# Expert slots: h turned by 32x32 block transposes over a DRAM exchange, second products two slots behind

## The chip, the core and the metric

One core of one Trainium2 chip runs the kernel in one launch. The metric is device time in microseconds (us), the median of the runs. The core has five engines with queues of their own: TensorE (matrix products and transposes, results in PSUM), VectorE, ScalarE, GpSimd and SyncE (SP), which here only issues DMA transfers. Engines wait for one another by semaphores.

## The reference

Attention with a cumulative bias gives x [4 x 576, 512]. Then comes the part that the change touches, a mixture of 8 experts with one expert per token, and a gated feed-forward layer with a short convolution.

```
logits = x @ w_gate;  e = argmax(logits)            # or the expert of the token before
h   = maximum(x[b, s] @ w1[e], 0.0)                 # 512 -> 1024
y   = p[e] * (h @ w2[e])                            # 1024 -> 512
h2  = maximum(y @ w_in, 0);  conv over 3 tokens;  out = (h2 * sigmoid(conv)) @ w_out
```

## The kernel before

`attention` runs first and takes about the first 200 us. A routing stage (`tensor_route`, `vector_route`, 200 to 219 us) sorts the 2304 tokens by expert into SLOTS = 25 slots of 128 tokens, each slot with tokens of one expert only. In this run the experts have 3, 2, 3, 3, 3, 2, 3 and the rest of the slots. Then the expert stage works slot by slot, from 219 to 529 us, and the last stage (w_in, convolution, w_out) follows.

Every product is taken in three parts, high x high, high x low and low x high (`PARTS`), where high is the value rounded to fp32r and low is what it leaves. So a slot's first product `hidden(s)` is 2 halves of 4 blocks of 3 parts, 24 matrix products on TensorE (L1289), into `h_bank` (wide_bank0, one PSUM bank for each half). The second, `output(s)`, is 8 blocks of 3 parts, 24 products too (L1306), into `y_bank` (row_bank0). An operand must have the summed dimension on the partitions. Hence x of the slot is turned by 4 TensorE transposes (`turn_x`, L1255) and moved from PSUM into high and low (`move_x`, VectorE, L1374 and L1376), and h is cut at zero (`relu`, L1382, into `h_sb`), turned by 8 TensorE transposes into `ht_bank` (wide_bank1; `turn_h`, L1327) and moved likewise into `h_tr` (`move_h`, L1392 and L1396). `move_y` (L1411) copies y to `y_sb`, and SP stores it to `y_sorted` in DRAM (L1206). There is one `y_bank`, one `h_sb`, one `xs_tr`, one `h_tr`, one `ht_bank`, and the semaphores guard them.

The order is written out by hand. TensorE's loop body is

```
hidden(s);  turn_x(s + 1);  output(s - 1);  turn_h(s)
```

and VectorE's is relu(s), move_x(s + 1), move_y(s - 1), move_h(s). The last slot is cut in halves: hidden(24, first half), output(23), turn_last, turn_h(24, first half), hidden(24, second half), output(24). `turn_last` makes 5 small transposes for placing the last slot's rows. Before a slot's products TensorE loads two numbers of the slot into registers (`weights_of`, L1271 and L1272): which half of the weight ring, and how many low parts must be ready.

The weight ring holds two experts. ScalarE issues the load of w1 of expert e when the first products of e - 2 are done, makes the high parts (L902), then issues w2 when the second products of e - 2 are done, and makes its high parts. GpSimd makes the low parts (L912) behind them. Before that, GpSimd gathers the rows of x of all 25 slots by indirect DMAs (L1164), two in flight.

## Time and profile before

| | us |
|---|---|
| median of 3 runs | 746.98 |
| lowest, highest | 746.82, 748.25 |
| span of the profiled execution | 746.1 |
| TensorE busy in it | 735.4 |
| VectorE busy in it | 432.8 |
| GpSimd busy | 329.1 |
| ScalarE busy | 322.1 |

The page of the profile gives the busy time of each engine, the load of each in 40 slices of 18.65 us, and the chain of work that ended last. The timeline merges like instructions in order of time. A row has the start and the length in us, then engine, line, operation, what it writes and reads, and the count; in brackets stands how long the engine was idle before it and what ended that. A matrix product's start is recorded, its end is modelled. A product's length (0.39 us) is therefore longer than the distance between two starts.

### The profile page before, as it was taken

The numbers are of one execution on the slowest core, as the hardware profiler recorded it, in microseconds if no ns is written. First come the engines' busy times: TensorE is split into PE (matmuls) and PEld (weight loads), VectorE is DVE, ScalarE is ACT, GpSimd is POOL, SyncE is SP. The second block draws the span as 40 slices with busy tenths as digits, with TensorE's granted clock in tenths as the row PEclk, the third lists the DMA queues.
The fourth block names the chain that finished last, engine by engine and source line by source line (L and its number), as shares of the span: only waits on it lengthen the run. The fifth ranks groups of instructions, "written<-read, shape, count | busy, mean of one in ns | idle before, by whom it ended". The sixth has DMA issues, their size and how long they took to land.

```text
span 746.1 us, 15123 instructions
## 1 busy us (share of the span) xinstructions
PE 735.4 (99%) x4971; PEld 626.7 (84%) x4971; DVE 432.8 (58%) x1042; ACT 322.1 (43%) x635; POOL 329.1 (44%) x442
## 2 busy tenths in 40 slices
PE   8999999999989999999999999999999999999998
PEld 6788887887887888888888888888899889889986
DVE  5777878878776544444444545454399455636510
ACT  5777878878430112212121311100397345535620
POOL 7759788887325469444444854400521100000000
PEclk9999999999999999999999999999999999999999
DMA  7888879984064666333334543200421110000011
GB/s 161 206 211 224 230 204 217 239 223 124 17 200 142 232 193 249 144 127 142 127 141 127 171 160 119 89 29 29 139 62 33 43 36 15 29 29 14 29 43 56
DMA packets 99848, 93.39 MB, mean 125 GB/s; under 512 B 62124, under 2 KB 71620, under 8 KB 99780
## 3 DMA queue, kind: packets, MB, share of 16 engines
q1 hardware_dynamic: 79252, 46.51, 22.9%
q10 hardware_dynamic: 17056, 34.69, 13.6%
q0 software_dynamic: 3472, 11.28, 5.3%
q8 instruction: 44, 0.72, 0.4%
q14 instruction: 24, 0.20, 0.1%
HBM read 76.13 MB, written 16.33 MB: 124 GB/s over the span
## 4 chain that ended last, share of the span: by engine, by line
PE 70%; DVE 1%; DMA 0%; issue 0%; ACT 0%; POOLq 0%; DVEq 0%; ACTq 0%
PE row_bank L1306 19%; PE wide_bank L1289 18%; PE wide_bank L1551 14%; PE row_bank L1589 13%; PE wide_bank L1327 3%; PE bank L1255 1%; PE bank L1520 1%; DMA x_slots<-x_rows,token_of 0%; PE bank L1540 0%; PE wide_bank L28 0%; PE row_bank L1540 0%; PE bank L1017 0%; DVE y_sb L1411 0%; DVE xs_tr L1376 0%; DVE xs_tr L1374 0%
## 5 line engine op out<-in xcount | busy, mean ns | idle before, releaser
L912 POOL TENSOR_TENSOR ring<-raw_w,ring 128x2048 fp32r<-128x2048 f32 x28 | 128.6, 4614 | 87.7 <-ACT ring L902 87.7
L1289 PE MATMUL wide_bank<-ring,xs_tr 128*128 x600 | 143.3, 394 | 0.7 <-DVE xs_tr L1368 0.4
L1306 PE MATMUL row_bank<-ring,h_tr 128*128 x600 | 143.5, 394 | 0.0
L902 ACT ACTIVATE ring<-raw_w 128x2048 fp32r<-128x2048 f32 x30 | 55.8, 1908 | 200.3 <-DMA raw_w<-in_moe_w_dram 169.6
L1306 PEld LDWEIGHTS row_bank<-ring,h_tr 128*128 128x128 f32 x600 | 110.8, 188 | 22.7
L1289 PEld LDWEIGHTS wide_bank<-ring,xs_tr 128*128 128x128 f32 x600 | 110.7, 188 | 22.9 <-issue 1.1
L1551 PE MATMUL wide_bank<-x_tr,ring 128*128 128x288 f32 x768 | 107.7, 297 | 0.0
L1551 PEld LDWEIGHTS wide_bank<-x_tr,ring 128*128 128x128 f32 x768 | 103.2, 188 | 0.9
L1589 PE MATMUL row_bank<-ring,g_tr 128*128 128x512 f32 x432 | 100.1, 389 | 0.0
L1589 PEld LDWEIGHTS row_bank<-ring,g_tr 128*128 128x128 f32 x432 | 80.5, 188 | 16.1
L692 ACT ACTIVATE prob<-score,row_min 128x128 f32<-128x128 f32 (+2 forms) x144 | 83.4, 580 | 17.9 <-DVE row_min L555 14.6
L251 POOL TENSOR_SCALAR bias<-ncum_row,cum_col 128x128 f32<-128x128 f32 (+3 forms) x128 | 67.2, 535 | 37.1 <-DVE row_min L555 31.9
L1641 DVE SCALAR_TENSOR_TENSOR conv<-h_pad,conv_col,conv 128x576 f32<-128x576 f32 x64 | 52.2, 816 | 53.9 <-ACT conv L1702 52.7
L555 DVE CUSTOM_DVE_ANT_0 score<-score_ps,bias 128x128 f32<-128x128 f32 (+2 forms) x144 | 69.2, 514 | 19.2 <-issue 13.3
L1411 DVE COPY y_sb<-row_bank 128x512 f32<-128x512 f32 x25 | 17.3, 694 | 98.8 <-PE row_bank L1306 98.8
L1382 DVE TENSOR_SCALAR h_sb<-wide_bank 128x512 f32<-128x512 f32 x48 | 33.2, 691 | 56.7 <-PE wide_bank L1289 56.0
L1493 POOL DMA_INDIRECT y_tok<-y_sorted,place_i x20 | 20.2, 1010 | 92.9 <-PE bank L1520 46.4
L361 PE MATMUL turn_ps<-identity,prob 128*128 128x128 f32 x320 | 50.1, 279 | 1.0 <-ACT tail_tr L709 0.6
L1164 POOL DMA_INDIRECT x_slots<-x_rows,token_of x25 | 26.0, 1041 | 49.1 <-DMA x_slots<-x_rows,token_of 24.1
L361 PEld LDWEIGHTS turn_ps<-identity,prob 128*128 128x128 f32 x320 | 36.4, 141 | 11.6 <-issue 5.0
L321 PE MATMUL score_ps<-k_tr,q_tr 64*128 64x128 f32 (+3 forms) x256 | 44.9, 469 | 0.1
L1693 ACT ACTIVATE h_pad<-wide_bank 128x576 f32<-128x576 f32 x32 | 20.9, 654 | 55.6 <-PE wide_bank L1551 55.5
(236 smaller groups left out, 1009.5 us busy)
## 6 DMA issues: line engine op xcount, KB each, us to landing
raw_w<-in_moe_w_dram ACTq DMA_DIRECT2D x12, 2048.0 KB, 8.8
ncum_row<-cum_rows SPq DMA_DIRECT2D x15, 512.0 KB, 5.6
y_sorted<-y_sb SPq DMA_DIRECT2D x26, 256.0 KB
raw_w<-in_moe_w_dram SPq DMA_DIRECT2D x12, 512.0 KB, 3.9
ncum_tail<-cum_rows SPq DMA_DIRECT2D x32, 144.0 KB, 4.4
out_dram<-out_sb ACTq DMA_DIRECT2D x18, 256.0 KB, 2.0
v_nat<-in_v_dram SPq DMA_DIRECT2D x32, 128.0 KB, 3.0
q_nat<-in_q_dram SPq DMA_DIRECT2D x30, 128.0 KB, 4.0
```

Source lines behind the costliest of these rows:

```text
L251: return nc.gpsimd.tensor_scalar(out, row, col, 1.0, ALU.add, ALU.mult)
L321: nc.tensor.matmul(out[:, hh, 0:(i + 1) * P], q_tr[u][at, i * P:(i + 1) * P], k_tr[u][at, 0:(i + 1) * P], start=True, stop=True).then_inc( ...
L361: last = nc.tensor.transpose(bank[:, at + j * P:at + (j + 1) * P], prob[unit(p, n) % 4][:, j * P:(j + 1) * P], identity[:, :])
L555: nc.vector.tensor_tensor_reduce(out=o, in0=a, in1=b, scale=1.0, scalar=3.0e38, op0=ALU.add, op1=ALU.min, accum_out=row_min[:, at % 4:at % ...
L692: nc.scalar.activation(prob[at % 4][:, 0:w], score[at % 3][:, 0:w], ACT.Exp, bias=row_min[:, at % 4:at % 4 + 1], scale=-1.0, accum_out=row ...
L902: nc.scalar.activation(high, whole, ACT.Copy).then_inc(high_ready, 1)
L912: nc.gpsimd.tensor_tensor(low, whole, high.bitcast(F32), ALU.subtract).then_inc(low_ready, 1)
L1289: last = nc.tensor.matmul(h_bank[:, half, :], xs_tr[:, a, kb, :], ring[:, bass.ds(n, 1), b, at:at + FH].rearrange("p a c -> p (a c)"), sta ...
L1306: last = nc.tensor.matmul(y_bank[:, :], h_tr[:, a, kb, :], ring[:, bass.ds(n, 1), 2 + b, kb * D:(kb + 1) * D].rearrange("p a c -> p (a c)" ...
L1551: last = nc.tensor.matmul(wide_bank[j % 2][:, half, 0:HALF], ring[:, 0, w, col:col + P], x2_tr[:, x, kb, at:at + HALF], start=kb == 0 and ...
L1589: last = nc.tensor.matmul(row_bank[outs % 2][:, :], g_tr[:, a, kb, lo:hi], ring[:, 0, 2 + w, kb * D:(kb + 1) * D], start=kb == 0 and (a, w ...
L1641: ins = V.scalar_tensor_tensor(c[:, :], h[:, k:k + S], conv_col[:, k * KF + f:k * KF + f + 1], c[:, :], ALU.mult, ALU.add)
```

## The change

Slots 2 to 23 are no longer turned by TensorE. VectorE's relu writes h to `h_sb` with the columns ordered so that each quarter of them (32 of every 128) lies together. SP writes `h_sb` to DRAM (`h_turn`), waits for it, and reads it back in four transfers, each of which takes one quarter of the columns to one quarter of the partitions, with the 128 tokens side by side (`h_exchange`). The buffer read into is `x_slots` of slots 0 to 3, used by then. VectorE turns the 32x32 blocks from there to `ht_bank` (`h_turned`), and makes high and low parts out of PSUM (`move_h_blocks`). Slots 0, 1 and 24 are turned by TensorE as before.

The second products run two slots behind the first. In the loop TensorE does hidden(s), turn_x(s + 1), output(s - 2). In four places the order differs: slots 2, 3 and 4 at the start, and the end. Each slot has a second need number of its own for w2, for which `vector_route` gets four more steps. ScalarE and GpSimd take the weights interleaved: w1 of e + 1, then w2 of e. Four gathers of x may be in flight. VectorE's, ScalarE's, GpSimd's and SP's loops are written out.

```diff
         nc.gpsimd.tensor_tensor(low, whole, high.bitcast(F32), ALU.subtract).then_inc(low_ready, 1)
 
-    def low_parts(pool, e, n):
...
+    def parts_upto(e, piece):
+        if e < 2:
+            return PIECES * e + piece + 1
+        if piece >= PIECES // 2:
+            return PIECES * e + PIECES - 1 + piece - (e == E) * (PIECES // 2)
+        return PIECES * e - 1 + piece + (e == 2) * (PIECES // 2)
+
+    def low_parts(pool, e, w):
+
+        for piece in (2 * w, 2 * w + 1):
+            low_part(pool, e, piece)
 
...
-        act.wait_ge(first_loaded[n], 16)
+        act.wait_ge(first_loaded[n // 2], 16 * (n % 2 + 1))
...
+            if part % 2:
+                sp.wait_ge(first_loaded[part // 2], 16)
...
+        then(V.tensor_scalar(slot_f[:, 3, :], slot_f[:, 1, :], 3.0, -float(PIECES // 2), ALU.is_ge, ALU.mult))
+        then(V.tensor_scalar(slot_f[:, 4, :], slot_f[:, 1, :], 2.0, float(PIECES // 2), ALU.is_ge, ALU.mult))
+        then(V.tensor_scalar(slot_f[:, 2, :], slot_f[:, 1, :], float(PIECES), float(PIECES), ALU.mult, ALU.add))
         then(V.tensor_scalar(slot_f[:, 1, :], slot_f[:, 1, :], float(PIECES), float(PIECES // 2), ALU.mult, ALU.add))
+        then(V.tensor_tensor(slot_f[:, 1:3, :], slot_f[:, 1:3, :], slot_f[:, 3:5, :], ALU.add))
         then(V.tensor_copy(free_i[:, :], tiles_upto[0:1, 1:1 + E]))
         dve.wait_ge(exps_ready, 1)
-        V.tensor_copy(slot_i[:, :, :], slot_f[:, :, :]).then_inc(slot_ready, 1)
+        V.tensor_copy(slot_i[:, :, :], slot_f[:, 0:3, :]).then_inc(slot_ready, 1)
...
-            above(pool, slot_loaded[s % 2], 16 * (s // 2))
+            above(pool, slot_loaded[s % GATHERS], 16 * (s // GATHERS))
             pool.indirect_dma_start(out=x_slots[:, s, :], out_offset=None, in_=x_rows,
-                                    in_offset=bass.IndirectOffsetOnAxis(ap=token_of[:, s:s + 1], axis=0)).then_inc(slot_loaded[s % 2], 16)
+                                    in_offset=bass.IndirectOffsetOnAxis(ap=token_of[:, s:s + 1], axis=0)).then_inc(slot_loaded[s % GATHERS], 16)
...
+    BY_PE = 2
+    h_swapped = [x_slots[:, 2 * n:2 * n + 2, :].rearrange("p s d -> p (s d)") for n in range(2)]
+    h_out, h_back, h_blocks, y_begun = sem("h_out"), sem("h_back"), sem("h_blocks"), sem("y_begun")
...
+    Q = 32
+    QUARTERS = P // Q
...
     def sync_experts(sp):
         sp.wait_ge(y_zero, 1)
         sp.dma_start(y_sorted[LAST:LAST + P, :], y_sb[:, :]).then_inc(last_zeroed, 16)
-        with sp.Fori(0, SLOTS - 1) as s:
+
+        def h_exchange(s):
+            n, i = s % 2, s - BY_PE
+            sp.wait_ge(h_ready, 2 * s + 2)
+            above(sp, h_back, 16 * QUARTERS * i)
+            sp.dma_start(h_turn[n], h_sb[:, :]).then_inc(h_out, 16)
+            sp.wait_ge(h_out, 16 * (i + 1))
+            if i >= 2:
+                sp.wait_ge(h_blocks, 2 * i - 2)
+            for g in range(QUARTERS):
+                sp.dma_start(h_swapped[n][g * Q:(g + 1) * Q, :].rearrange("p (i c) -> p i c", i=QUARTERS),
+                             h_turn[n][:, g * F // QUARTERS:(g + 1) * F // QUARTERS].rearrange("(i r) c -> r i c", r=Q))\
+                    .then_inc(h_back, 16)
+
+        def y_store(s):
             sp.wait_ge(y_ready, s + 1)
-            sp.dma_start(y_sorted[bass.ds(s * P, P), :], y_sb[:, :]).then_inc(y_stored, 16)
+            sp.dma_start(y_sorted[s * P:(s + 1) * P, :], y_sb[:, :]).then_inc(y_stored, 16)
+
+        y_store(0)
+        h_exchange(2)
+        y_store(1)
+        h_exchange(3)
+        h_exchange(4)
+        for s in range(2, SLOTS - 1):
+            y_store(s)
+            if s + 3 < SLOTS - 1:
+                h_exchange(s + 3)
 
         for t in range(TB):
             sp.wait_ge(gathered[t], 16)
...
 
     def scalar_experts(act):
 
-        def next_weights(e, n, i, first, second):
-            slots = act.value_load(free_i[0:1, bass.ds(e - 2, 1)], min_val=1, max_val=SLOTS)
-            act.wait_ge(h_done, 2 * slots)
-            load_weights(act, n, 0, first)
-            high_parts(act, n, i, 0)
-            act.wait_ge(y_done, slots)
-            load_weights(act, n, 1, second)
-            high_parts(act, n, i, 1)
+        def slots_upto(e):
+            return act.value_load(free_i[0:1, e:e + 1], min_val=1, max_val=SLOTS)
+
+        def first_matrix(e):
+            act.wait_ge(h_done, 2 * slots_upto(e - 2))
+            load_weights(act, e % 2, 0, w1[e] if e < E else w_in)
+
+        def second_matrix(e):
+            act.wait_ge(y_done, slots_upto(e - 2))
+            load_weights(act, e % 2, 1, w2[e] if e < E else w_out)
 
         high_parts(act, 1, 0, 1)
 
@@ -1227,12 +1272,15 @@
             act.wait_ge(h_done, half + 1)
             nc.scalar.activation(h_sb[:, half * FH:(half + 1) * FH], h_bank[:, half, :], ACT.Relu).then_inc(h_ready, 1)
         act.wait_ge(slot_ready, 1)
-        with act.Fori(1, E // 2) as i:
-            for n in range(2):
-                e = 2 * i + n
-                next_weights(e, n, i, w1[bass.ds(e, 1)].rearrange("a d f -> (a d) f"),
-                             w2[bass.ds(e, 1)].rearrange("a f d -> (a f) d"))
-        next_weights(E, 0, E // 2, w_in, w_out)
+        first_matrix(2)
+        high_parts(act, 0, 1, 0)
+        for e in range(2, E):
+            first_matrix(e + 1)
+            second_matrix(e)
+            high_parts(act, (e + 1) % 2, (e + 1) // 2, 0)
+            high_parts(act, e % 2, e // 2, 1)
...
-        low_parts(pool, E, 0)
+        low_parts(pool, 2, 0)
+        for e in range(2, E):
+            low_parts(pool, e + 1, 0)
+            low_parts(pool, e, 1)
+        low_parts(pool, E, 1)
+
...
+    h_by_quarter = h_sb[:, :].rearrange("p (g k c) -> p g k c", g=QUARTERS, k=KF)
+
+    def quarters_of_half(half):
+        return h_by_quarter[:, :, half * HK:(half + 1) * HK, :].rearrange("p g k c -> p k g c")
...
             last.then_inc(xs_turned, 1)
 
-        def weights_of(s, more):
-
-            need = pe.value_load(slot_i[0:1, 1, bass.ds(s, 1)], min_val=PIECES // 2, max_val=PIECES * E)
+        def weights_of(s, w):
+
+            need = pe.value_load(slot_i[0:1, 1 + w, bass.ds(s, 1)], min_val=PIECES // 2, max_val=PIECES * (E + 1))
             n = pe.value_load(slot_i[0:1, 0, bass.ds(s, 1)], min_val=0, max_val=1)
-            pe.wait_ge(low_ready, need + more)
+            pe.wait_ge(low_ready, need)
             return n
 
         def hidden(s, halves=range(2), loaded=None):
@@ -1293,7 +1347,7 @@
                 last.then_inc(h_done, 1)
 
         def output(s, blocks=range(KF), loaded=None, ends=False):
-            n = weights_of(s, PIECES // 2) if loaded is None else loaded
+            n = weights_of(s, 1) if loaded is None else loaded
             if s == 0:
                 pe.wait_ge(conv_ready, 1)
...
                 last.then_inc(y_done, 1)
 
...
         n = weights_of(1, 0)
         turn_h(0)
-        for s in range(1, SLOTS - 1):
-            hidden(s, loaded=n if s == 1 else None)
-            turn_x(s + 1, (s + 1) % 2, (s + 1) // 2)
-            output(s - 1)
-            turn_h(s)
+        hidden(1, loaded=n)
+        turn_x(2)
+        output(0)
+        turn_h(1)
+        hidden(2)
+        turn_x(3)
+        output(1)
+        hidden(3)
+        turn_x(4)
+        for s in range(4, SLOTS - 1):
+            hidden(s)
+            turn_x(s + 1)
+            output(s - 2)
 
         s = SLOTS - 1
         hidden(s, (0,))
+        output(s - 2)
+        turn_last()
         output(s - 1)
-        turn_last()
         turn_h(s, (0,))
         hidden(s, (1,))
-        n = weights_of(s, PIECES // 2)
+        n = weights_of(s, 1)
         output(s, range(2), n)
         turn_h(s, (1,))
...
 
+        def h_turned(s):
+            dve.wait_ge(h_back, 16 * QUARTERS * (s - BY_PE + 1))
+            for half in range(2):
+                dve.wait_ge(ht_ready, 2 * s + (half - 1))
+                V.transpose(ht_bank[:, half, :].rearrange("p (k i r) -> p k i r", k=HK, i=QUARTERS),
+                            h_swapped[s % 2].rearrange("p (i k c) -> p k i c", i=QUARTERS, k=KF)[:, half * HK:(half + 1) * HK, :, :])\
+                    .then_inc(h_blocks, 1)
+
+        def move_h_blocks(s, halves=range(2)):
+            for half in halves:
+                if s == SLOTS - 2 and half == 0:
+                    dve.wait_ge(y_begun, 1)
+                else:
+                    dve.wait_ge(y_done, s)
+                blocks = slice(half * HK, (half + 1) * HK)
+                turned = ht_bank[:, half, :].rearrange("p (k c) -> p k c", k=HK)
+                dve.wait_ge(h_blocks, 2 * (s - BY_PE) + (1 + half))
+                V.tensor_copy(h_tr[:, 0, blocks, :], turned).then_inc(ht_high, 1)
+                dve.wait_ge(ht_high, 2 * s + (1 + half))
+                V.tensor_tensor(h_tr[:, 1, blocks, :], turned, h_tr[:, 0, blocks, :].bitcast(F32), ALU.subtract).then_inc(ht_ready, 1)
+
         def relu(s, halves=range(2)):
             for half in halves:
                 dve.wait_ge(h_done, 2 * s + (1 + half))
-                above(dve, ht_turned, 2 * s + (half - 1))
-                V.tensor_scalar(h_sb[:, half * FH:(half + 1) * FH], h_bank[:, half, :], 0.0, None, ALU.max)\
-                    .then_inc(h_ready, 1)
+                if s > BY_PE:
+                    dve.wait_ge(h_out, 16 * (s - BY_PE))
+                else:
+                    above(dve, ht_turned, 2 * s + (half - 1))
+                to, of = h_sb[:, half * FH:(half + 1) * FH], h_bank[:, half, :]
+                if BY_PE <= s < SLOTS - 1:
+                    to, of = quarters_of_half(half), of.rearrange("p (k g c) -> p k g c", k=HK, g=QUARTERS)
+                V.tensor_scalar(to, of, 0.0, None, ALU.max).then_inc(h_ready, 1)
 
         def move_h(s, halves=range(2)):
...
         dve.wait_ge(last_zeroed, 16)
-        with dve.Fori(1, SLOTS - 1) as s:
+        for s in range(1, SLOTS - 1):
+            if s >= 4:
+                h_turned(s - 2)
+                move_h_blocks(s - 2)
+            if s == 3 or s > 4:
+                move_y(s - 3 if s > 4 else 1)
             relu(s)
             move_x(s + 1)
-            move_y(s - 1)
-            move_h(s)
+            if s == 1:
+                move_y(0)
+                move_h(1)
+        h_turned(SLOTS - 3)
+        move_h_blocks(SLOTS - 3)
+        move_y(SLOTS - 4)
         relu(SLOTS - 1, (0,))
         V.tensor_scalar(last_row[:, :], place_i[:, 0:TB], -1.0, float(LAST), ALU.mult, ALU.add).then_inc(last_placed, 1)
         dve.wait_ge(last_placed, 1)
@@ -1431,6 +1531,10 @@
             rows = slice(0, TAIL if t == TB - 1 else P)
             V.tensor_scalar(last_nat[rows, t, :], back[rows, :], last_row[rows, t:t + 1], weight[rows, t:t + 1], ALU.is_equal, ALU.mult)\
                 .then_inc(last_made, 1)
+        h_turned(SLOTS - 2)
+        move_h_blocks(SLOTS - 2, (0,))
+        move_y(SLOTS - 3)
+        move_h_blocks(SLOTS - 2, (1,))
         move_y(SLOTS - 2)
         move_h(SLOTS - 1, (0,))
```

Routing on VectorE, the steps between the slot count's reduction and slot_i, before:

```order
L1120 TENSOR_TENSOR slot_w<-slot_w,sign_row 1x25x7
L1122 TENSOR_REDUCE slot_f<-slot_w 1x25
L1123 TENSOR_SCALAR slot_f<-slot_f 1x25
L1124 CAST free_i<-tiles_upto 1x8
L1126 CAST slot_i<-slot_f 1x50
L1129 TENSOR_SCALAR token_of<-row_bank 128x17
```

and in the changed kernel:

```order
L1130 TENSOR_TENSOR slot_w<-slot_w,sign_row 1x25x7
L1132 TENSOR_REDUCE slot_f<-slot_w 1x25
L1133 TENSOR_SCALAR slot_f<-slot_f 1x25
L1134 TENSOR_SCALAR slot_f<-slot_f 1x25
L1135 TENSOR_SCALAR slot_f<-slot_f 1x25
L1136 TENSOR_SCALAR slot_f<-slot_f 1x25
L1137 TENSOR_TENSOR slot_f<-slot_f 1x50
L1138 CAST free_i<-tiles_upto 1x8
L1140 CAST slot_i<-slot_f 1x75
L1143 TENSOR_SCALAR token_of<-row_bank 128x17
```

Four small steps stand in the same chain ahead of slot_i.

On TensorE, between the second products of slot 0 or a later one and the first products of the next slot but one (names: wide_bank<-identity,h_sb is turn_h, row_bank<-ring,h_tr is output, wide_bank<-ring,xs_tr is hidden), before:

```order
L1306 ISA
L1306 MATMUL row_bank<-ring,h_tr 128x512 x2
L1327 MATMUL wide_bank<-identity,h_sb 128x128 x8
L1271 TENSOR_LOAD slot_i
L1271 ISA x2
L1272 TENSOR_LOAD slot_i
L1272 ISA x2
L1289 ISA
```

and between output(2) and hidden(5) of the changed kernel:

```order
L1360 ISA
L1360 MATMUL row_bank<-ring,h_tr 128x512 x2
L1325 TENSOR_LOAD slot_i
L1325 ISA x2
L1326 TENSOR_LOAD slot_i
L1326 ISA x2
L1343 ISA
L1343 MATMUL wide_bank<-ring,xs_tr 128x512
```

The eight transposes are gone, and the register loads stand right behind the second products. Between the first products of slots 3 and 4 there is now this:

```order
L1343 MATMUL wide_bank<-ring,xs_tr 128x512
L1343 ISA
L1343 MATMUL wide_bank<-ring,xs_tr 128x512 x2
L1309 MATMUL bank<-identity,x_slots 128x128 x4
L1325 TENSOR_LOAD slot_i
L1325 ISA x2
L1326 TENSOR_LOAD slot_i
L1326 ISA x2
L1343 ISA
L1343 MATMUL wide_bank<-ring,xs_tr 128x512
```

No second products lie between them. On VectorE, one turn of the loop before, from the relu on:

```order
L1382 TENSOR_SCALAR h_sb<-wide_bank 128x512
L1380 REGISTER_ALU
L1382 TENSOR_SCALAR h_sb<-wide_bank 128x512
L1371 REGISTER_ALU
L22 ISA
L1374 CAST xs_tr<-bank 128x512
L1376 TENSOR_TENSOR xs_tr<-bank,xs_tr 128x512
L22 ISA
L1411 COPY y_sb<-row_bank 128x512
L1392 CAST h_tr<-wide_bank 128x512 x2
L1396 TENSOR_TENSOR h_tr<-wide_bank,h_tr 128x512 x2
```

and of the changed kernel, slot 5:

```order
L1447 STREAM_TRANSPOSE wide_bank<-x_slots 128x512 x2
L1460 CAST h_tr<-wide_bank 128x512
L1462 TENSOR_TENSOR h_tr<-wide_bank,h_tr 128x512
L1460 CAST h_tr<-wide_bank 128x512
L1462 TENSOR_TENSOR h_tr<-wide_bank,h_tr 128x512
L1502 COPY y_sb<-row_bank 128x512
L1474 TENSOR_SCALAR h_sb<-wide_bank 128x4x4x32 x2
L1439 CAST xs_tr<-bank 128x512
L1441 TENSOR_TENSOR xs_tr<-bank,xs_tr 128x512
```

The parts of h now come first, from two block transposes, and the y copy moves ahead of the relu. On SP, from y store to y store in the loop of the changed kernel (before, each loop turn had the y store alone):

```order
L1239 DMA y_sorted<-y_sb 128x512
L1228 DMA h_turn<-h_sb 128x1024
L1233 DMA x_slots<-h_turn 32x4x256 x4
L1239 DMA y_sorted<-y_sb 128x512
```

Five transfers of the exchange lie between two y stores.

## Rows read from the trace of the kernel before

**Rows 1.** Page: engine busy; DMA in tenths of 40 slices; chain by engine.

```profile
PE 735.4 (99%) x4971; PEld 626.7 (84%) x4971; DVE 432.8 (58%) x1042; ACT 322.1 (43%) x635; POOL 329.1 (44%) x442
...
DMA  7888879984064666333334543200421110000011
...
PE 70%; DVE 1%; DMA 0%; issue 0%; ACT 0%; POOLq 0%; DVEq 0%; ACTq 0%
```

**Rows 2.** Timeline of one slot, TensorE and VectorE (start, length, engine, line).

```profile
301.31 0.39 PE L1306 MATMUL row_bank<-ring,h_tr 128*128 x1
...
301.54 1.03 PE L1327 MATMUL wide_bank<-identity,h_sb 128*128 128x128 f32 x8
...
302.33 5.71 PE L1289 MATMUL wide_bank<-ring,xs_tr 128*128 x24
302.44 1.28 DVE L1392 CAST h_tr<-wide_bank 128x512 fp32r<-128x512 f32 x2
...
307.88 0.60 PE L1255 MATMUL bank<-identity,x_slots 128*128 128x128 f32 x4
308.07 0.69 DVE L1382 TENSOR_SCALAR h_sb<-wide_bank 128x512 f32<-128x512 f32 x1 [1.94 <-PE wide_bank L1289]
...
308.23 5.74 PE L1306 MATMUL row_bank<-ring,h_tr 128*128 x24
308.68 0.68 DVE L1374 CAST xs_tr<-bank 128x512 fp32r<-128x512 f32 x1
309.40 0.69 DVE L1376 TENSOR_TENSOR xs_tr<-bank,xs_tr 128x512 fp32r<-128x512 f32 x1
...
313.81 1.03 PE L1327 MATMUL wide_bank<-identity,h_sb 128*128 128x128 f32 x8
314.10 0.69 DVE L1411 COPY y_sb<-row_bank 128x512 f32<-128x512 f32 x1 [4.01 <-PE row_bank L1306]
```

**Rows 3.** Routing: timeline, then the register load's own row (durations, first and last start).

```profile
216.78 0.17 DVE L1123 TENSOR_SCALAR slot_f<-slot_f 1x25 f32<-1x25 f32 x1
216.98 0.43 DVE L1124 CAST free_i<-tiles_upto 1x8 int32<-1x8 f32 x1
...
217.44 0.18 DVE L1126 CAST slot_i<-slot_f 1x50 int32<-1x50 f32 x1
...
219.32 0.63 PE L1264 MATMUL bank<-identity,x_slots 128*128 128x128 f32 x4 [1.15 <-DMA x_slots<-x_rows,token_of]
...
L1271 PEldq TENSOR_LOAD <-slot_i x51: 298/302/487, 217.7 to 519.9; - x51
```

**Rows 4.** Timeline of the last slot and the start of the next stage.

```profile
510.86 2.98 PE L1289 MATMUL wide_bank<-ring,xs_tr 128*128 x12
...
513.68 5.61 PE L1306 MATMUL row_bank<-ring,h_tr 128*128 x24
...
530.03 0.69 DVE L1411 COPY y_sb<-row_bank 128x512 f32<-128x512 f32 x1 [3.24 <-PE row_bank L1306]
...
530.78 1.56 PE L1540 MATMUL bank<-last_at,y_sb 128*128 128x384 f32 x4
```

**Rows 5.** Page, DMA issues (KB each, us to landing); an issue's own time on SP (ns).

```profile
ncum_row<-cum_rows SPq DMA_DIRECT2D x15, 512.0 KB, 5.6
...
out_dram<-out_sb ACTq DMA_DIRECT2D x18, 256.0 KB, 2.0
...
q_nat<-in_q_dram SPq DMA_DIRECT2D x30, 128.0 KB, 4.0
...
L1206 SPq DMA_DIRECT2D y_sorted<-y_sb x24: 332/332/376, 241.4 to 520.2; - x24
```

**Rows 6.** Weights: a load's landing, the high part (page), expert 2's first low parts.

```profile
DMA to landing us min/median/max: 7.7/8.8/12.0
...
L902 ACT ACTIVATE ring<-raw_w 128x2048 fp32r<-128x2048 f32 x30 | 55.8, 1908 | 200.3 <-DMA raw_w<-in_moe_w_dram 169.6
...
267.38 9.17 POOL L912 TENSOR_TENSOR ring<-raw_w,ring 128x2048 fp32r<-128x2048 f32 x2
```

41 lines of the change are left out of this document (21 added, 20 removed).

## The prediction

> **What bounds the kernel now.** I read the page's busy line first: TensorE is busy for 735.4 of 746.1 us, and the chain that ended last is TensorE work for 70% of the span, with 1% of VectorE [rows 1]. So time is taken out only by taking TensorE work out, or put in by making TensorE wait. Next I read one slot of the expert stage in the timeline [rows 2]. Its order on TensorE is 24 first products (L1289), 4 transposes of the next x (L1255), 24 second products of the slot before (L1306), 8 transposes of h (L1327), and no row shows an idle time before a TensorE group. The h transposes begin at 301.54 and at 313.81: a slot takes 12.27 us. VectorE's seven pieces follow TensorE (4.01 us idle before the y copy, 1.94 before a relu), so VectorE has room.
>
> **What the transposes cost.** The last second product starts at 301.31, the next first product at 302.33, which is 1.02 us [rows 2]. Products in a row start every (5.71 - 0.39) / 23 = 0.231 us. Without the eight transposes the next product would start at 301.54, so they cost 1.02 - 0.23 = 0.79 us a slot. The change takes them from slots 2 to 23, 22 slots: **-17.4 us**. Two checks on it. First, the register loads of a slot number, which now stand right between products, might come out from behind the transposes. At the last slot's half this boundary exists already: 12 products from 510.86 that end at 13.84, with the second products from 513.68, one pitch after the last start at 13.45 [rows 4]. So nothing comes out. Second, if each new boundary costs 0.04 more, the term is 16.5; if weight loads overlap better than the start times say, it may be up to 20. I take 17.4. A new slot takes 12.27 - 0.79 = 11.48 us.
>
> **Routing.** Four more VectorE steps stand before slot_i is written: three scalar steps and one addition, in a chain of waits. Such a step starts 0.20 us before the next one (216.78 to 216.98 [rows 3]), so slot_i comes 0.8 us later. The first register load on TensorE starts at 217.7, right behind slot_i's end (217.44 plus its 0.17), and TensorE's first work waits until 219.32 [rows 3]. That row names the gather of x as the releaser, which would hide the 0.8. But the two loads with their register steps fill the time between, so I take it whole: **+0.8** (bounds 0 and 0.8). The SP waits on half pieces (first_loaded) stand behind loads issued a head pair earlier, and cost nothing.
>
> **Start of the new order.** Slots 3 and 4 have their first products back to back; only 4 transposes of x(4) lie between. In a normal slot the x move is covered by second products: relu's second half at 308.07, cast at 308.68, subtraction from 309.40 for 0.69, over at 310.09 [rows 2]. PE would be ready at 308.23. A release is seen about 0.06 later (a copy from 530.03 for 0.69, its reader at 530.78 [rows 4]). So hidden(4) waits 310.15 - 308.23 = **+1.9**, once. Bounds 1.5 and 2.5.
>
> **The slot loop.** I follow VectorE from the start of hidden(s), t = 0. The y_done of the slot before is seen at 0.29 (313.81 to 314.10 [rows 2]). Then cast, subtract, cast, subtract: starts 0.72 apart inside a half (308.68 to 309.40) and 0.60 between halves (1.28 for two casts of 0.68), so 2.64 until the y copy starts, at 2.93, and 3.62 when it ends. TensorE needs h_tr and the y bank at 5.9. Relus end at 4.3 and 6.4, the x move at 7.8. The two block transposes of the next h must fit before 11.48 + 0.29, and as much later as the y copy has slack (5.9 - 3.7 = 2.2): 6.2 us for two, 3.1 each. No row shows a block transpose. The nearest is a VectorE piece of the same 128x512, 0.68 to 0.69 us [rows 2]; I take 0.7, bounds 0.4 and 4 times that, 2.8. All of these are under 3.1, so the price is **0**. The Trainium skill (Vector Engine (DVE) Microarchitecture Reference, 3.8 The reshape front-end and per-opcode configuration) says that the transpose array sustains one element per cycle per lane, which is also what a piece of 0.69 us for 512 elements looks like; the sum would be the same.
>
> **The exchange.** Per slot SP writes h to DRAM (512 KB), waits, and issues four reads of 128 KB. No row has it, so I bound it. Write: between the 2.0 us of a 256 KB store and the 5.6 of a 512 KB transfer in the busy attention stage; reads: four issues of 0.3 to 0.6 and a last landing of 3 to 4.0 [rows 5]. Together 6.3 to 11.4, and I take 8. One exchange starts only when the one before is back, so the cycle must be below 11.48, and even the upper bound is. Latency: relu ends at 6.4, the blocks are needed by transposes that must start by 2 x 11.48 + 1.1 = 24.1, so 17.7 us are there for 8 to 11.4. h_sb is free for the next relu when the write has landed, 6.4 + 2 to 5.6 = 8.4 to 12, and that relu starts at 15.2. Price **0**. Two things are queued on SP behind the exchange's waits: the y store of the slot three before and the next exchange. The exchange has issued its last read by 6.4 + 5.6 + 1.8 = 13.8, and the next y copy ends at 11.48 + 3.6 = 15.1, so the store doesn't wait.
>
> The Trainium skill (VectorE: DVE Perf Modes, The three transpose paths) speaks against this change: VectorE transposes only 32x32 blocks, TensorE is advised for 128x128, and a plain DMA that makes a transpose by strides is called 19 times slower than the crossbar. Here the DMA moves runs of 256 elements (1 KB) and leaves the inside of a block to VectorE. If the rule held in spite of that, the exchange would take far more than a slot and the time would be that of the slower rival below, and beyond.
>
> **Weights.** A pair of loads, w1 of expert e+1 and w2 of e, now starts when the first products of e-1 are done. One load lands in 7.7 to 12.0 us, a high part takes 1.9, and two low parts take GpSimd 9.2 [rows 6]. With the median of 8.8 the second load of a pair lands at 17.6 and its first high part is there at 19.5; GpSimd has worked on the first matrix from 10.7 to 19.9 and is done with the second at 29.1. w2(e) is needed 5.9 + 2.5 slots later, 34.7 us after the issue: 5.5 us of slack. Expert 2's first parts are tighter: GpSimd ended them at 267.4 + 9.2 = 276.6 [rows 6], and slot 5's first products began two slots before 302.33, at 277.8. Now these are due near 272.2 + 0.8. The parts stood behind the gathers of x, which were held to two in flight; with four they end earlier, and the parts can start when their high halves are there, about 258, and end at 267. Price **0**, but it is the thinnest cover, with a DMA that is already busy by 4 to 7 tenths in this stage [rows 1] and gets 1 MB more per slot.
>
> **End.** From t0 = start of the last slot's first half: VectorE ends y copy 21 at 3.62 as above, and output(22) starts at 3.68, where output(23) now starts at 513.68 - 510.86 = 2.82 [rows 4]: +0.86. Then output(23) must wait for the y copy of slot 22: 0.29 + 0.69 + 0.06 = 1.04 us, in which the five small transposes of turn_last now run. Before, those five stood behind output(23). Taking them away there gives back some 0.6, if nothing else is late; but the first products of the next stage need tiles of y that are gathered after slot 23's store, and behind them TensorE waits for the last y copy anyway (530.03 to 530.78 [rows 4]). I credit 0.1. So 0.86 + 1.04 - 0.1 = **+1.8** (1.2 to 1.9).
>
> **Sum.** -17.4 + 0.8 + 1.9 + 1.8 = -12.9 on the profiled span of 746.1: 733.2. The median of the runs lies 0.9 above the span, so **734.1**.
>
> **Rivals.**
> (a) *Weights late.* If the two loads of a pair share the DMA engines with exchanges, and w2 lands more than 5.5 us late, each of six experts stalls TensorE by the excess: 1 to 2 us each gives 6 to 12, so 737 (few) to 746. For it: the loads are back to back and the DMA gets busier. Against: even in its busiest slices here the DMA is at 6 tenths, and the load's median of 8.8 us already holds some company. 17%.
> (b) *The exchange becomes the bound, slower than before.* Its cycle (write, landing, four reads, landing, next write) takes more than 11.48 us. The slack of some 8 us is eaten first, and then each of 21 slots takes the cycle's time. At 13 us: 21 x 1.52 - 8 = 24 us, 758. It turns to slower when the mean cycle passes 11.48 + (12.9 + 8) / 21 = 12.5 us. For it: my upper bound is 11.4 without a weight load beside it. Against: 512 KB need only 1 or 2 us of transfer, and a store of half the size is over in 2.0. With a block transpose of over 3.4 us as another way to the same end: 10%.
> (c) *No change* (the blocks work but TensorE waits 0.6 us in each slot): 745 to 749, 3%.
> (d) *Better*: the 0.8 of routing is hidden, the end costs 1.2, or the removed transposes are worth 0.9 each: 730 to 732. 8%.
> The forecast itself, 732 to 737: 62%.
>
> **How the numbers follow.** 0.2% (1.5 us) is about what a measurement of this kernel can tell from no change. Faster takes forecast, (d) and all but a little of (a): 0.86; same 0.03; slower 0.11. The range reaches from (d) at 731 into (a) at 741, and leaves out some 2 in 10: (b), (c), and the upper half of (a).
>
> **What would show it.** Right: TensorE's groups repeat every 11.5 us; one idle of 1.9 us before the first products of slot 4, with the x move as releaser; idles of 0.9 and 0.5 (1.04 less the transposes that run in it) before the last two second products; the block transposes at 0.7 us; TensorE starts 0.8 later in the expert stage. Wrong: idle time before second products in each slot, released by VectorE's h_tr whose transposes wait for a DMA (b), or by GpSimd's low parts every third slot (a). If the slot period is 12.27 still, the transposes' price was mis-sized.

## Result, and the profile after

Median 742.18 us (738.27 to 745.16, 6 runs) against 746.94 (746.51 to 748.25, 6 runs) of the kernel before: ratio 0.9935, 95% interval 0.9913 to 0.9957. Here the change makes the kernel faster, but by 4.8 us and not by the 12.9 forecast, and the time lies above the range. On two other chips it makes it slower (third and fourth group). The profiled span is 740.8 (before 746.1).

Page of after: busy line, DMA in tenths, chain by engine, then two groups (busy, mean ns, idle before them).

```profile
PE 718.6 (97%) x4795; PEld 609.1 (82%) x4795; DVE 462.8 (62%) x1090; ACT 321.4 (43%) x634; POOL 328.2 (44%) x442
...
DMA  8888889894076876677687777731521100000011
...
PE 64%; DMA 5%; DVE 2%; issue 2%; SPq 0%; POOL 0%; ACT 0%; POOLq 0%; DVEq 0%; ACTq 0%
...
L1360 PE MATMUL row_bank<-ring,h_tr 128*128 x600 | 144.7, 397 | 7.3 <-issue 4.0
...
L1447 DVE STREAM_TRANSPOSE wide_bank<-x_slots 128x512 f32<-128x512 f32 x44 | 28.9, 703 | 43.6 <-DMA x_slots<-h_turn 43.4
```

Against [rows 1], TensorE has 17 us less work but is idle more; DMA, absent from the chain before, is 5% of it; the DMA engines stand mostly at 6 to 8 tenths in the expert stage instead of 3 to 6. A block transpose takes 0.70 us, and VectorE waits 43.4 us for what they read.

Timeline of TensorE in a slot in which nothing is late:

```profile
288.93 5.60 PE L1343 MATMUL wide_bank<-ring,xs_tr 128*128 x24
294.37 0.60 PE L1309 MATMUL bank<-identity,x_slots 128*128 128x128 f32 x4
294.73 5.71 PE L1360 MATMUL row_bank<-ring,h_tr 128*128 x24
300.28 1.98 PE L1343 MATMUL wide_bank<-ring,xs_tr 128*128 x8
```

The slot takes 11.35 us, and the four slots from 288.93 on take 11.36 on average, 0.91 less than the 12.27 of [rows 2]: 22 times 0.91 is 20.0. So the work taken out is worth more than forecast, and waits and slower products took 15 us back. The largest are in this part of the chain of waits (start, us, what):

```profile
248.38 9.49 DMA h_turn<-h_sb
...
259.47 2.88 DMA x_slots<-h_turn
262.41 4.09 DMA h_turn<-h_sb
...
267.83 9.41 DMA x_slots<-h_turn
```

The timeline of the same stretch has two weight loads, issued by ScalarE, and what came behind the late reads:

```profile
247.66 0.37 ACTq L891 DMA_DIRECT2D raw_w<-in_moe_w_dram  x1
...
259.51 3.72 ACT L903 ACTIVATE ring<-raw_w 128x2048 fp32r<-128x2048 f32 x2 [30.92 <-DMA raw_w<-in_moe_w_dram]
...
266.98 6.28 ACTq L891 DMA_DIRECT2D raw_w<-in_moe_w_dram  x2
...
277.10 3.71 ACT L903 ACTIVATE ring<-raw_w 128x2048 fp32r<-128x2048 f32 x2 [13.88 <-DMA raw_w<-in_moe_w_dram]
277.27 1.32 DVE L1447 STREAM_TRANSPOSE wide_bank<-x_slots 128x512 f32<-128x512 f32 x2 [8.06 <-DMA x_slots<-h_turn]
...
281.13 0.68 DVE L1502 COPY y_sb<-row_bank 128x512 f32<-128x512 f32 x1
282.03 4.34 PE L1360 MATMUL row_bank<-ring,h_tr 128*128 x12 [3.29 <-DVE y_sb L1502]
```

A load is issued at 247.66 and its high part begins at 259.51; the exchange's write, issued 0.7 behind it, lands at 257.9. The next load is issued at 266.98 and is there at 277.10; the reads, issued from 266.52 on, are there at 277.24. In this trace seven of the 22 writes take 6.3 to 9.5 us, and each was issued 0.7 to 4.4 us behind a load; the other 15 take 2.7 to 4.5. With a load and the exchange under way together, in the two stretches above, the DMA engines had no room left (start:end and length, then busy us and count of TensorE, its weight load, VectorE, ScalarE and GpSimd, then the granted clock, the busy share of the DMA engines and GB/s):

```profile
252.00:258.00 6.00, 6.00 (x28) 4.99 (x27) 0.72 (x2) 0.00 (x0) 0.00 (x0) 1.00 1.00 398
272.00:277.00 5.00, 5.00 (x24) 4.13 (x22) 0.00 (x0) 0.00 (x0) 0.00 (x0) 1.00 1.04 351
```

So a write or read that starts beside a 2 MB load lands about when the load does. Then VectorE needs 4.5 us for two transposes, four parts and the y copy (277.27 to 281.81), and TensorE has waited 3.29 us.

### The profile page after: what moved, and what is told of

Read it like the earlier page. It is cut to its first block, busy times and chain, and to the rows that moved or that the text cites. A ratio compares the mean times of both kernels' runs of the same rounds, so it can differ in the third digit from the quotient of the medians.

```text
span 740.8 us, 14655 instructions
## 1 busy us (share of the span) xinstructions
PE 718.6 (97%) x4795; PEld 609.1 (82%) x4795; DVE 462.8 (62%) x1090; ACT 321.4 (43%) x634; POOL 328.2 (44%) x442
## 4 chain that ended last, share of the span: by engine, by line
PE 64%; DMA 5%; DVE 2%; issue 2%; SPq 0%; POOL 0%; ACT 0%; POOLq 0%; DVEq 0%; ACTq 0%
PE row_bank L1360 17%; PE wide_bank L1343 16%; PE wide_bank L1655 14%; PE row_bank L1693 13%; DMA h_turn<-h_sb 2%; DMA x_slots<-h_turn 2%; PE bank L1309 1%; PE bank L1624 1%; DMA y_tok<-y_sorted,place_i 1%; DMA x_slots<-x_rows,token_of 0%; SPq L1233 0%; DMA y_sorted<-y_sb 0%; PE wide_bank L28 0%; PE bank L1644 0%; POOL y_tok L1597 0%
## 5 line engine op out<-in xcount | busy, mean ns | idle before, releaser
L1343 PEld LDWEIGHTS wide_bank<-ring,xs_tr 128*128 128x128 f32 x600 | 113.4, 190 | 27.3 <-issue 4.1
L1447 DVE STREAM_TRANSPOSE wide_bank<-x_slots 128x512 f32<-128x512 f32 x44 | 28.9, 703 | 43.6 <-DMA x_slots<-h_turn 43.4
L1460 DVE CAST h_tr<-wide_bank 128x512 fp32r<-128x512 f32 x44 | 29.9, 681 | 26.7 <-PE row_bank L1360 26.7
L442 PEld LDWEIGHTS turn_ps<-prob_tr,v_nat 128*64 128x64 f32 x640 | 34.6, 137 | 12.2 <-issue 12.2
```

The lines of the kernel that those rows point to most:

```text
L442: last = nc.tensor.matmul(bank[at, at_q:at_q + P], v_nat[p % 2][:, j, at], prob_tr[i][:, hh, j * P:(j + 1) * P], start=j == 0, stop=j == i)
L1343: last = nc.tensor.matmul(h_bank[:, half, :], xs_tr[:, a, kb, :], ring[:, bass.ds(n, 1), b, at:at + FH].rearrange("p a c -> p (a c)"), sta ...
```

## Experiments

The first four ran on one chip, where the kernel before takes 747.83 us (746.6 to 748.15). **a1_again** is the changed kernel, unaltered.

> The changed kernel unaltered, as the yardstick for the others of this job. Both theories: 738 to 745 us as before, with TensorE's slot period at 11.35 us, waits of 0.2 to 1.2 us in front of some second products, and 3 to 4 us in front of output(3).

743.54 us (740.90 to 744.06), ratio 0.9951 [0.9934, 0.9967]: the result again. In its trace the long wait isn't in front of output(3) but in front of output(4), 1.98 us: which slot is hit, and how hard, differs between runs of one kernel, whose times spread over 3 to 7 us where the kernel before spreads over 2.

**a3_small_exchange** moves a quarter of the exchange's bytes, with the same number of transfers and the same waits; three quarters of h are left out, so the output isn't the reference's.

```
-  sp.dma_start(h_turn[n], h_sb[:, :])
+  sp.dma_start(h_turn[n][0:Q, :], h_sb[0:Q, :])
   ...                                  # and each read 32 rows x 256 instead of 32 x 4 x 256
```

> The exchange writes 32 of the 128 rows of h and reads them back, a quarter of the bytes with as many transfers; products of slots 2 to 23 get wrong values for three quarters of their tokens, so part of the computation is left out. Theory A (waiting on the exchange's transfers beside weight loads is the cause): the loads land in about 9 us again, no wait on the exchange in the loop, only the fixed ones (1.9 at slot 4, 1.3 at the end, routing) stay: 731 to 735. Rival C (what is lost is not bandwidth but the latency of transfers queued behind a weight load's, which a quarter of the bytes doesn't shorten): 738 or more, with landings over 6 us still there beside a load.

733.45 us (732.50 to 733.64), ratio 0.9809 [0.9793, 0.9826], 10.1 less than a1. DMA issues of a3 from 256 to 540 us (KB each, median us to landing), then those of after in the same stretch:

```profile
raw_w<-in_moe_w_dram ACTq DMA_DIRECT2D x11, 2048.0 KB, 10.0
...
x_slots<-h_turn SPq DMA_DIRECT2D x88, 32.0 KB, 1.8
h_turn<-h_sb SPq DMA_DIRECT2D x21, 128.0 KB, 2.5
```

```profile
raw_w<-in_moe_w_dram ACTq DMA_DIRECT2D x11, 2048.0 KB, 11.4
x_slots<-h_turn SPq DMA_DIRECT2D x88, 128.0 KB, 3.0
h_turn<-h_sb SPq DMA_DIRECT2D x21, 512.0 KB, 3.1
```

With a quarter of the bytes the time is near the 734.1 that I had forecast (by luck in part, since the transposes were worth more and routing cost more), and of TensorE's waits in the slots only those at fixed places are left (hidden(4), the end). So the missing gain is in the bytes of the exchange beside the loads (with them the packets are a quarter too; no run separates the two). The typical landing was short before as well, 3 us; what went is the length of the long ones, at most 7.0 us for a write and 6.1 for a read here, 9.5 and 9.4 in after. Landings of over 6 us are left, as the rival had said, but TensorE waits for none of them.

**a2_y_first** puts the y copy ahead of the parts of the next slot on VectorE; **a4_first_slot_by_constant** lets the first slot wait for its weights by a constant, so that slot_i isn't in its path.

```
         for s in range(1, SLOTS - 1):
+            if s == 3 or s > 4:
+                move_y(s - 3 if s > 4 else 1)
             if s >= 4:
                 h_turned(s - 2)
                 move_h_blocks(s - 2)
-            if s == 3 or s > 4:
-                move_y(s - 3 if s > 4 else 1)
             ...                                        # likewise for slot 21 behind the loop
```

```
-        pe.wait_ge(slot_ready, 1)
-        n = weights_of(0, 0)
         turn_first_x()
+        pe.wait_ge(low_ready, PIECES // 2)
+        n = 0
         ...
+        pe.wait_ge(slot_ready, 1)                      # ahead of slot 1's numbers
```

> VectorE copies y of the slot before ahead of the block transposes and the parts of h, instead of behind them; nothing else moves. Theory A (late landing of the exchange reaches TensorE through the y copy that is queued behind the block transposes): the waits of 0.2 to 1.2 us in the loop and the 0.9 at the last slot go, output(3) waits 1.4 less, so 4 to 6 us less than the changed kernel, 736 to 738. Rival B (TensorE waits for weight parts that are late, since the loads now land in 11.5 instead of 8.8 us): no effect, within 1 us.

740.58 us (736.51 to 741.23), ratio 0.9891 [0.986, 0.9921]. TensorE's waits by line (us in total, times, longest):

```profile
PE row_bank L1360 <- DVE h_tr L1462: 4.3, 4, 2.8
```

3.0 us less than a1, with four runs each whose ranges just touch, and not the 4 to 6 expected. The waits are not gone, they have another releaser: the copy no longer stands behind late transposes, but the second products need their parts as well. And the parts come late in a new way. The copy may overwrite `y_sb` only when the y store before has landed, SP issues that store behind the reads of the exchange, and now the transposes stand behind the copy. In a2 VectorE waits 40.7 us for the store, in 7 pieces; the piece ahead of the longest wait of TensorE, from the chain of waits:

```profile
396.04 10.49 DMA y_sorted<-y_sb
```

So a 256 KB store beside the loads becomes late as well (3.0 us at the median in after). e1 and e2 have this wait too, with 55.1 and 31.5 us.

> TensorE takes slot 0's two numbers as constants (slot 0 is always expert 0's), so it no longer waits for slot_i before slot 0, only before slot 1. Theory A (the four steps lengthen TensorE's idle time ahead of slot 0 from 1.15 to 1.75 us, and the granted clock falls for 12 products, 1.5 us): the idle time falls to about 0.4 us, the 12 products take 3.0 instead of 4.5, together 2 to 3 us less than the changed kernel. Rival D (the low clock there has nothing to do with the idle time): only 1 us less, products still at 4.5.

741.00 us (740.51 to 741.20), ratio 0.9912 [0.9896, 0.9929], 2.5 less than a1. The first slot on TensorE, in after and in a4:

```profile
218.81 0.63 PE L1318 MATMUL bank<-identity,x_slots 128*128 128x128 f32 x4 [1.75 <-issue]
...
220.29 4.48 PE L1343 MATMUL wide_bank<-ring,xs_tr 128*128 x12 [0.40 <-DVE xs_tr L1433]
```

```profile
218.05 0.66 PE L1318 MATMUL bank<-identity,x_slots 128*128 128x128 f32 x4 [0.54 <-DMA x_slots<-x_rows,token_of]
...
219.46 3.02 PE L1343 MATMUL wide_bank<-ring,xs_tr 128*128 128x512 f32 x12 [0.31 <-DVE xs_tr L1434]
```

Of the 2.5 us, the shorter idle time (0.54 instead of 1.75) is 1.2. The rest is that behind 1.75 us of idle time the same twelve products take 4.48 us instead of 3.02.

**A second group, on another chip** (before: 747.28, 746.33 to 749.37). b1 holds back the load of w1(3) until the exchange of slot 3 is back, b2 splits the output of slot 1 around hidden(3), b3 issues each 2 MB load as four of 512 KB with two in flight, and b4 has a2, a4, b2 and b3 in one.

```
+            if e == 2:                                  # b1
+                act.wait_ge(h_back, 16 * QUARTERS * 2)
             first_matrix(e + 1)
```

```
-        output(1)                                       # b2
+        n = weights_of(1, 1)
+        output(1, range(HK), n)
         hidden(3)
         turn_x(4)
+        output(1, range(HK, KF), n)
         ...                                            # SP: y store of slot 1 behind exchange(3)
```

> The changed kernel, with one wait more: ScalarE issues w1 of expert 3 (and behind it w2 of expert 2) only when the exchange of slot 3 is back. Theory E (an exchange transfer issued beside a weight load lands about when the load does, so it's the load under way, not the exchange's own bytes, that costs): the reads of slot 3's exchange land in 3 to 4 instead of 6 to 9 us, the wait of 2 to 3.5 us in front of output(3) and the clock loss behind it fall to under 1 in sum; 2 to 4 us less than the changed kernel (743.5): 739 to 741.5. Rival F (these reads are slow by their 1 KB runs in one quarter of the partitions): no effect.

> output(1) is cut in halves, one ahead of hidden(3) and one behind turn_x(4), so that hidden(3) and hidden(4) are no longer back to back; SP stores y of slot 1 behind the exchange of slot 3. Theory A: the wait in front of hidden(4), 1.8 to 2.1 us, goes and nothing takes its place; if the exchange of slot 3 still ends when the weight load does, part of it moves to output(3). 0 to 2 us less than the changed kernel: 741.5 to 743.5.

> ScalarE issues each weight matrix in four DMAs of 512 KB with at most two under way, instead of one of 2 MB with a second behind it; bytes, order of the matrices and everything else stay. Theory E (transfers wait behind what a load has queued): exchange writes and reads beside a load land in at most 5 to 6 us instead of 9 to 10, the waits in the loop and at output(3) go; 4 to 8 us less than the changed kernel: 735.5 to 739.5. Rival G (the DMA engines lack bandwidth for the bytes of both): landings stay at 8 to 10 us beside a load, time at 742 or more, or weights come late and TensorE waits for GpSimd's parts.

> y copy first, slot 0 by constants, output(1) split, loads in quarters. If the effects add up (3.0, 2.5, 2 and 4 to 8 us, less what y first and the quarters share): 729 to 733, under the kernel with the quarter-sized exchange (733.5), which kept the other waits.

b1 757.35 us (756.28 to 758.96), b2 757.65 (756.85 to 758.71), b3 750.00 (748.04 to 752.98), b4 749.15 (745.33 to 751.63): all slower than the kernel before (b3 by 0.3%, b4 by 0.2%), which I had not expected. b3 is still 7.4 us below b1. b2's timeline has the new cause, first VectorE and then TensorE:

```profile
238.15 0.69 DVE L1476 TENSOR_SCALAR h_sb<-wide_bank 128x512 f32<-128x512 f32 x1
252.54 0.69 DVE L1476 TENSOR_SCALAR h_sb<-wide_bank 128x512 f32<-128x512 f32 x1 [13.71 <-remote]
```

```profile
248.99 0.37 PE L1383 MATMUL wide_bank<-identity,h_sb 128*128 128x128 f32 x1 [1.80 <-issue]
```

Between two relus of slot 1, whose products had long ended, VectorE stands for 13.7 us with no instruction as the releaser ("remote"), and TensorE meanwhile issues one transpose in some 2 us. The gathers of x run back to back until 252. Whether this came with the edits or with the chip only the unaltered kernel could tell.

**Third group, a third chip** (before: 746.96, 746.07 to 748.45). c1 is the changed kernel, c2 is b1's edit again, c3 has two gathers in flight instead of four (`GATHERS = 2`), c4 has a2's and a4's edits.

> The changed kernel unaltered. In the last job four variants of it all had a stretch of 13 to 16 us from 238 us on in which VectorE had no instruction to run (its wait is put down to no engine and no data transfer), TensorE's transposes came one every 2 us, and one page of instructions was fetched in 245 to 260 us instead of 230 to 245, behind the gathers of x. Theory H (it depends on the chip or on the run's surroundings, and the kernel is open to it since its loops are written out and four gathers queue up): this kernel has it too if hold has it here, 755 to 758. Rival I (it's in the altered code of those four): this kernel takes 741 to 745 and has no such stretch, whatever hold does.

> The same kernel as the one held back in the last job (one wait of ScalarE more). Theory H: as the unaltered kernel of this job, less 2 to 4 us if the weight load's company is what the exchange of slot 3 waits for. Rival I: 757 again, 13 us above the unaltered one.

> The changed kernel with two gathers of x in flight instead of four, as in the kernel before. Theory H: no stretch without instructions in any state, since a page fetch waits behind two gathers at most; if the unaltered kernel takes 757 here, this one takes 745 or less. The price of it, by the trace of the kernel before: gathers end near 267 instead of 248, GpSimd's first low parts of expert 2 end near 277 instead of 271, and slot 5 waits for them 2 to 4 us: 743 to 747 where the unaltered one is undisturbed.

> y copy first and slot 0's numbers as constants together; four gathers. If the two effects add up (3.0 and 2.5 us) and the stretch doesn't occur: 737.5 to 739. With the stretch: 750 to 753.

c1 754.18 us (752.66 to 756.43): **the unaltered kernel is slower than before on this chip**, ratio 1.0095 [1.0068, 1.0123], with a wait for "remote" of 14.2 us. So the stretch belongs to the change and the chip (or what else its neighbours did to the memory), and not to the edits of b. c2 754.09 (753.63 to 755.17): no effect, but it tests little. Behind the stretch of 14 us the exchange of slot 3 comes ahead of the load anyway: in c1 its reads are issued at 278.97 and the load at 282.10, in c2 the held load at 283.16. The case that the edit was to prevent didn't occur, here and in b1. c4 749.71 (747.07 to 756.04): 4.5 less than c1, where a2 and a4 took 5.5 off on the first chip; the waits for "remote" come in shorter pieces, the longest 5.4. c3 747.99 (746.33 to 751.70): the stretch is gone, 6.2 us less than c1, but still 0.2% above the kernel before and above the 745 expected. TensorE's waits by line in c3 name what replaced it:

```profile
PE wide_bank L1343 <- POOL ring L913: 7.6, 1, 7.6
```

The last gather is issued at 270.08 instead of 247.05, GpSimd's low parts of expert 2 stand behind it, and TensorE waits 7.6 us for these.

**Fourth group, a fourth chip** (before: 746.98, 25 runs). d1 is the changed kernel; d2 keeps four in flight but puts the gathers of slots 14 and up behind the low parts of expert 2.

```
-        gather_slots(pool, 8, SLOTS)
+        gather_slots(pool, 8, 14)
         low_parts(pool, 2, 0)
+        gather_slots(pool, 14, SLOTS)
```

> The changed kernel unaltered, the yardstick of this chip. If the chip is like that of the first group: 741 to 744 us and no idle time of VectorE over 4 us before 257 us. If it is like those of the second and third: 752 to 757 us, with about 14 us of VectorE's idle time in the first slots that the trace ascribes to no instruction.

> The gathers of x for the slots from 14 on are issued behind GpSimd's low parts of the first matrix of expert 2 instead of ahead of them. Theory (the gathers, back to back until 248 us, hold up something that the first slots need): the 14 us stretch is gone, and the time is 741 to 744 us on any chip; on a chip without the stretch nothing changes by over 1.5 us. Rival (the stretch has nothing to do with the gathers, and two gathers in flight removed it by other timing): the time stays that of d1.

d1 756.53 us (752.73 to 758.22), with the stretch (14.9 us). d2 753.70 (752.20 to 755.45): the stretch is gone, so it hangs on the gathers that run beside it; yet the time falls by 2.8 only, with ranges that overlap. A "remote" wait of 5.3 us at slot 0's x move is left (4.6 in d1), where the first gathers run, and TensorE waits 3.7 us behind it. d2's timeline, TensorE:

```profile
301.64 4.63 PE L1361 MATMUL row_bank<-ring,h_tr 128*128 x10 [5.76 <-DVE y_sb L1503]
```

The moved gathers now run beside the exchange of slot 4 and a pair of loads: the last of its reads lands after 12.8 us, and TensorE waits 5.8. My expectation of 741 to 744 was wrong: I had counted the gathers' new place as free.

d3 is d2 with the edits of a2, a4 and b2; d4 is d3 without that of b2.

> d2 with three edits more: the y copy ahead of the parts of the next slot (2 to 3 us less on the first chip), the first slot's wait against a constant (2.5 us less), and the output of slot 1 split around hidden(3), so that TensorE has work while the exchange of slot 3 lands (3 to 4 us of its wait of 3.3 and of the slower clock behind it). Theory: the three losses stand one behind the other and add up: 734 to 737 us. Rival (the exchange of slot 3, which lands with the weight load whatever is issued ahead, only moves the wait to hidden(4)): 738 to 740 us.

> d3 without the split of the output of slot 1. Theory: 3 to 4 us more than d3, 737 to 740 us. Rival: the same as d3 within 1 us, since the split only moves the wait.

d3 748.07 us (746.16 to 754.24), d4 750.14 (747.80 to 753.30), 11 and 10 us above what the theory gave. The split is worth 2.1, less than the 3 to 4 expected, with ranges that overlap; TensorE still waits 10.1 us for parts in d3.

**Fifth group, a fifth chip** (before: 747.67, 746.41 to 748.51). e1 is d3 with the gathers of slots 14 to 17 behind the low parts of expert 3's first and 2's second matrix, and the others behind the next pair. e2 is e1 with the loads in quarters, as b3.

```
+            for k, (e, w, q) in enumerate(parts):      # e2: parts are quarters of the matrices
+                if k >= 2:
+                    landed(begun[0] + k - 2)           # two transfers of 512 KB in flight
+                ...
+                quarter(e, w, q, begun[0] + k)
+                if k >= 2:
+                    high_of(*parts[k - 2])             # behind every second one that has landed
```

> d3 with the gathers of slots 14 to 17 behind the low parts of expert 3 and the second matrix of 2, and of the others behind the next pair. Theory (the gathers beside the exchanges of slots 3 to 5 made TensorE wait 10.1 us for parts in d3): half or more of that wait goes, 740 to 743 us. Rival (the weight loads alone make those landings long, as on the first chip): 745 to 748 us, as d3.

> e1 with each 2 MB weight load issued as four of 512 KB, two in flight. In the earlier group the quarters took 7.5 us off. Theory (an exchange issued beside a whole load lands with it): the waits for the exchange go, 735 to 739 us. Rival (with quarters the weights come later and TensorE waits for high parts, as 3 us or more in the waits): no better than e1.

e1 744.44 us (740.25 to 749.18, 10 runs), ratio 0.9969 [0.9944, 0.9994]; **e2 735.70 (732.39 to 739.88, 4 runs), ratio 0.9862 [0.9812, 0.9913]**, in the range expected; e1 lies 1.4 above its own. Waits of TensorE by line in e1, then in e2, e2's DMA issues from 256 to 540 us, and one of those from 332 to 344:

```profile
PE row_bank L1362 <- DVE h_tr L1467: 9.5, 4, 4.9
```

```profile
PE row_bank L1380 <- DVE h_tr L1485: 3.5, 2, 3.1
```

```profile
raw_w<-in_moe_w_dram ACTq DMA_DIRECT2D x44, 512.0 KB, 5.6
h_turn<-h_sb SPq DMA_DIRECT2D x21, 512.0 KB, 4.0
x_slots<-h_turn SPq DMA_DIRECT2D x84, 128.0 KB, 3.9
```

```profile
h_turn<-h_sb SPq DMA_DIRECT2D x1, 512.0 KB, 10.8
```

With quarters the typical landing of the exchange is longer (4.0 and 3.9 instead of 3.1 and 3.0 in after), but those beside a load are shorter: in e1 seven writes take 6.4 to 10.4 us, in e2 four take 6.3 to 6.9 and one 10.8. That one runs beside the gathers that were moved there (GpSimd issues seven of them from 330.12 to 341.92) as well as beside a load, as does the 10.4 of e1. Behind it come the reads and the y store, and 3.1 of the 3.5 us of waits that are left. So quarters cure what the loads did, and the gathers are a second cause of the same kind.

The profiled span of e2 is 730.8. e2 beats the kernel before on its chip. It is a version for inputs like this one: by the code, the gathers placed late would wait for low parts that wait for them if the first two experts filled more than 14 slots (no run has such an input). The unaltered kernel didn't run on this chip, and neither e1 nor e2 shows a "remote" wait, so how much of the step from d3 to e1 is the chip stays open, and so does what e2 would do on a chip with the stretch. e2 against e1 is on one chip, 8.7 us, with ranges that don't meet.

## Why the prediction was wrong, point by point

**The removed transposes** were sized at 0.79 us a slot and are worth 0.91, 20.0 us in all instead of 17.4. That is case (d)'s reading of them. The 0.79 is the gap that they fill. What was left out is that the first products behind them also ran longer: from their start to the turn of x it was 5.55 us in [rows 2] (302.33 to 307.88), and it is 5.44 now (288.93 to 294.37).

**The exchange** is the step that failed. I bounded its cycle at 11.4 us, wrote that even this was below 11.48, and priced it at 0. The bounds came from transfers of [rows 5] in other stages, with no 2 MB load of this stage beside them. (They also count four issues at the low end and three at the high end; with four the high end is 12.0, already over 11.48. And the DMA engines were busy by 3 to 6 tenths in this stage, not 4 to 7: an average over 18.65 us, which hides what a load does. In the kernel before they are busy by 0.73 from 308.2 to 315.9 us, with a load, and by 0.05 from 316 to 326, without one.) Typical cycles were as taken (3.1 + 1.8 + 3.0, about 8), and rival (b) as worded, a *mean* cycle over 12.5, didn't come. But a mean isn't what TensorE waits for. Beside a load a cycle was 14 to 15 us (9.49 + 1.6 + 2.88; 4.09 + 1.3 + 9.41). The latency I gave it (17.7 us) doesn't hold in the start, where slots 2 and 3 are closer together, nor in the loop, where one late cycle also delays the next one. VectorE's waits from 256 to 545 us (total, times, longest) and one case in the loop:

```profile
DVE wide_bank L1447 <- DMA x_slots<-h_turn: 43.4, 11, 8.1
...
DVE h_sb L1474 <- DMA h_turn<-h_sb: 10.5, 5, 3.7
```

```profile
359.18 1.32 DVE L1447 STREAM_TRANSPOSE wide_bank<-x_slots 128x512 f32<-128x512 f32 x2 [5.80 <-DMA x_slots<-h_turn]
...
363.94 2.35 PE L1360 MATMUL row_bank<-ring,h_tr 128*128 x9 [0.81 <-issue]
```

In the loop TensorE's idle times (0.81, 0.61, 0.65 and 1.22) come to 3.3 us. Measured from start to start they cost 4.7, since a modelled end lies behind the time at which the next product could have started; the granted clock is 1.00 from 302 to 500 us, so none of it is slower products. At output(3) the start comes 3.5 late, and the slower products behind it add 1.35, together 4.9. So the exchange cost 9.6 us where the sum had 0; a3, with a quarter of the bytes, gives 10.1 back, and e2 8.7 against e1. I had noticed that the y copy was queued behind the parts and computed its slack with the transposes on time; a2 puts that queue place at 3.0 us.

**The slower products** were in no term. Two stretches of after (the granted clock is the last number but two), then hidden(4) in after and in d2:

```profile
220.30:222.30 2.00, 2.00 (x5) 1.69 (x6) 1.97 (x3) 0.00 (x0) 1.63 (x2) 0.50 0.71 211
282.00:284.00 2.00, 1.97 (x5) 1.59 (x6) 0.27 (x1) 0.35 (x1) 2.00 (x2) 0.50 0.36 142
```

```profile
261.23 5.72 PE L1343 MATMUL wide_bank<-ring,xs_tr 128*128 x24 [1.82 <-issue]
```

```profile
265.39 7.33 PE L1344 MATMUL wide_bank<-ring,xs_tr 128*128 x24 [1.82 <-issue]
```

Behind idle times of 1.75 and 3.29 us the granted clock stands at 0.50 of its full level (1.2 of 2.4 GHz) before it rises again: 12 products take 4.48 us instead of 3.0, and 24 take 7.06 instead of 5.71. But the same 1.82 us of idle time ahead of hidden(4) cost nothing in eight traces (after, a1, a3, b1, b3, c1, c3, d1: 5.7 to 5.8 us) and 1.6 us in four (c2, c4, d2, d4: 7.3 to 7.4), and behind 3.15 us 24 products took 5.71 in e1 and 7.34 in e2. So the length of the wait alone doesn't decide it, and what else does no run here shows.

**Routing** was put at +0.8 and came to +2.1: 0.6 of wait and 1.5 of slower products. The gather didn't hide the wait, as I had chosen. a4 takes 2.5 out of the path.

**Start of the new order**: +1.9 forecast, 1.82 of idle time and 2.1 from start to start measured. **End**: +0.86 and +1.04 less what runs inside it; the timeline has 0.88 and 0.31, and 0.57 at y_tok. Together that is +1.8 (2.0 from start to start), but the forecast had no wait for y_tok and counted more for the second one, so the match is luck in part.

```profile
501.91 5.75 PE L1360 MATMUL row_bank<-ring,h_tr 128*128 x24 [0.88 <-issue]
...
508.61 3.71 PE L1360 MATMUL row_bank<-ring,h_tr 128*128 x15 [0.31 <-issue]
```

**Weights**, rival (a), didn't happen as told: a load's median rose from 8.7 to 11.4 us in this stretch, but TensorE never waited for a weight part in after. It was close: expert 2's first parts end at 270.7 (forecast 267), 2.0 us ahead of hidden(5), and in c3 they were 7.6 us late. The collision was seen, with the wrong victim: above all it was the exchange that came late, and not the load.

**VectorE**: a block transpose takes 0.70 us, as taken, about as long as a cast of the same shape (0.68). The Trainium skill (Vector Engine (DVE) Microarchitecture Reference, 3.8 The reshape front-end and per-opcode configuration) has the transposing array sustain one element per cycle per lane. The trace doesn't speak against it, but with one size only it doesn't show a rate either. The rule of 19 times in the Trainium skill (VectorE: DVE Perf Modes, The three transpose paths) holds, by its own words, for a large innermost stride at the destination. The exchange has none, it writes runs of 1 KB: a read of 128 KB lands in 3.0 us, against 4.0 for a plain one of another stage in [rows 5]. So the rule neither applied nor was tested.

**The sum by the runs**, from start to start: -20.0 (transposes), +2.1 (routing), +2.1 (hidden(4)), +4.9 (output(3)), +4.7 (loop), +0.2 (the slots of hidden(2) and hidden(4)), +2.0 (end), -1.1, because the stages ahead ended 1.1 us earlier in this profile, and -0.2 in the last stage: -5.3, as the spans give.

**Open.** What VectorE fetched or waited for in the "remote" stretch is argued and not shown. In the 15 us from 230 on the trace of after has one transfer of 0.02 MB on the instruction queue beside the gathers, which b2 has only in the 15 us from 245 on, when the stretch ends:

```profile
q8 instruction: 1, 0.02, 0.5%
```

```profile
q8 instruction: 1, 0.02, 0.4%
```

That fits instructions which come late behind four gathers in flight. Shown is only that the stretch goes with the place and number of the gathers (c3, d2). Whether the loops that are now written out have a part in it no run tests. Why three chips have it and the first doesn't isn't known; and that the change is a gain of 4 to 5 us in the result and in a1, and a loss of 7 to 10 on two other chips is part of its result.

## What to carry to other kernels

Bound a new transfer by its landing beside the largest transfer that can be in flight with it, not by the typical one: a wait is set by the longest landing. Cutting the 2 MB loads into quarters with two in flight took the waits from 9.5 to 3.5 us and 8.7 us off the kernel. On an in-order engine put what the bound engine needs first ahead of work that waits for a DMA. And run a change that adds transfers on more than one chip before believing it.

## What the runs showed of the hardware

- A write of 512 KB that lands in 3.2 us at the median (2.7 at the least) took 9.5 us beside a 2 MB load, and reads of 128 KB 9.4 instead of 3.0: both ended about with the load, with the DMA engines busy for 1.00 and 1.04 of the time. With the loads in quarters the medians were 4.0 and 3.9 us, and the writes beside a load alone took 6.9 at most; beside a load and gathers one took 10.8.
- TensorE at a granted clock of 0.50 behind 3.29 us of idle time, and in the 2 us of products behind 1.75; at 1.00 in the slots, behind idle times of up to 1.22 us too. Behind 1.82 us 24 products took 7.3 us instead of 5.7 in four traces of twelve.
- With four gathers in flight, a wait of VectorE of 12 to 16 us in the first slots that the trace puts down to no instruction, in seven of the eight traces with the gathers in place on three chips (in the eighth, c4, it came in pieces), and in none of the four on the first chip nor in the result, while the kernel before took 747 to 748 us on all of these chips. The granted clock of 216 to 256 us in after and in b2:

```profile
216.00:256.00 40.00, 37.27 (x178) 30.65 (x177) 21.98 (x39) 4.91 (x4) 24.46 (x25) 0.96 0.74 209
```

```profile
216.00:256.00 40.00, 26.12 (x117) 19.98 (x115) 15.42 (x30) 4.87 (x4) 22.54 (x25) 0.82 0.61 163
```
